# Pair loads on SP wait for earlier pair loads, and pair 0's block sums stand one slot later

## The reference

```python
k_sum = k.reshape(B, H, nb, block, D).max(axis=3)
v_sum = v.reshape(B, H, nb, block, D).mean(axis=3)
scores_l = scale * np.matmul(q, k.transpose(0, 1, 3, 2))      # kept where |i - j| < 16
scores_s = scale * np.einsum('bhsd,bhnd->bhsn', q, k_sum) + np.log(block)
a = softmax over both; return np.matmul(a, np.concatenate([v, v_sum], axis=2))
```

## Time and profile before

| What | Value |
|---|---|
| Median of 3 runs | 351.02 us (348.58 to 351.9) |
| Profiled execution, whole time | 350.21 us |
| Profiled execution, span | 348.3 us |
| PE busy | 337.7 us, 97% of the span |
| PE weight loads busy | 304.0 us, 87% |
| DVE, ACT, POOL busy | 61%, 35%, 34% |
| Data moved | 24.72 MB, mean 71 GB/s |
| Mean granted clock of PE | 0.99 |

### The profile page before, as it was taken

The page is one execution under the profiler, slowest core; times in us unless marked ns, Lnnn a source line. Parts: engine busy times, 40 slices in busy tenths (PEclk is TensorE's granted clock), DMA queues, the critical chain, the costliest instruction groups (busy, mean ns, idle before and its releaser), DMA issues.

```text
span 348.3 us, 7109 instructions
## 1 busy us (share of the span) xinstructions
PE 337.7 (97%) x2886; PEld 304.0 (87%) x2886; DVE 211.6 (61%) x503; ACT 123.2 (35%) x364; POOL 117.6 (34%) x130
## 2 busy tenths in 40 slices
PE   7879799999999999999999999999999999999996
PEld 6768688888998899889999999998999999999984
DVE  5658678434309990363447984688656667766652
ACT  3667677756233132451111124221222232222212
POOL 6557668856609999400004920000000000000000
PEclk9989899999999999999999999999999999999999
DMA  7999738000212200163000200000000004000004
GB/s 245 291 313 236 212 122 289 2 2 3 64 58 93 105 0 2 48 203 114 0 0 2 60 0 3 0 2 0 0 2 0 0 2 181 0 2 0 0 3 181
DMA packets 9024, 24.72 MB, mean 71 GB/s; under 512 B 1184, under 2 KB 1184, under 8 KB 8992
## 3 DMA queue, kind: packets, MB, share of 16 engines
q1 hardware_dynamic: 8992, 24.26, 22.4%
HBM read 21.11 MB, written 3.15 MB: 70 GB/s over the span
## 4 chain that ended last, share of the span: by engine, by line
PE 92%; DMA 2%; POOL 2%; issue 1%; ACT 1%; DVE 1%; SPq 0%; POOLq 0%; DVEq 0%
PE bank L799 26%; PE bank L800 26%; PE bank L801 26%; PE bank L791 4%; PE bank L778 3%; PE bank L758 3%; DMA vw<-in_vw 2%; PE bank L849 1%; PE bank L768 1%; POOL vw L393 1%; ACT P L505 1%; POOL P L421 1%; PE bank L852 1%; DMA out<-obuf 1%; PE bank L884 1%
## 5 line engine op out<-in xcount | busy, mean ns | idle before, releaser
L801 PE MATMUL bank<-g_h,W_l 128*128 128x384 f32 x128 | 43.0, 336 | 0.0
L800 PE MATMUL bank<-g_l,W_h 128*128 128x384 f32 x128 | 42.9, 335 | 0.0
L799 PE MATMUL bank<-g_h,W_h 128*128 128x384 f32 x128 | 42.9, 335 | 0.0
L505 ACT ACTIVATE P<-P,nmax 128x120 f32<-128x120 f32 x96 | 36.7, 384 | 15.5 <-DVE nmax L634 15.3
L801 PE MATMUL bank<-wo_h,hg_l 128*128 128x512 f32 x96 | 38.0, 396 | 0.0
L800 PE MATMUL bank<-wo_l,hg_h 128*128 128x512 f32 x96 | 38.0, 396 | 0.0
L799 PE MATMUL bank<-wo_h,hg_h 128*128 128x512 f32 x96 | 37.9, 395 | 0.0
L801 PE MATMUL bank<-wsT_h,vn_l 128*128 128x384 f32 x96 | 32.1, 334 | 0.0
L799 PE MATMUL bank<-wsT_h,vn_h 128*128 128x384 f32 x96 | 32.1, 334 | 0.0
L800 PE MATMUL bank<-wsT_l,vn_h 128*128 128x384 f32 x96 | 32.1, 334 | 0.0
L421 POOL TENSOR_TENSOR P<-P,rinv 128x480 f32<-128x480 f32 x24 | 23.6, 986 | 23.8 <-DVE rinv L622 23.4
(11 more groups left out here) (111 smaller groups left out, 798.0 us busy)
## 6 DMA issues: line engine op xcount, KB each, us to landing
vw<-in_vw SPq DMA_DIRECT2D x16, 288.0 KB, 6.1
kT<-in_k SPq DMA_DIRECT2D x8, 384.0 KB, 5.4
qT<-in_q SPq DMA_DIRECT2D x8, 384.0 KB, 6.4
out<-obuf SPq DMA_DIRECT2D x12, 256.0 KB, 2.0
stage<-in_wsT SPq DMA_DIRECT2D x6, 384.0 KB, 3.2
stage<-in_w SPq DMA_DIRECT2D x4, 512.0 KB, 3.5
stage<-in_wo SPq DMA_DIRECT2D x4, 512.0 KB, 3.5
wi_most<-in_w_in SPq DMA_DIRECT2D x3, 512.0 KB, 12.0
```

The source lines that it names most:

```text
L505: a.activation(P[:, i % NP_, j, :], P[:, i % NP_, j, :], ACT.Exp, bias=nmax[:, c:c + 1], scale=-1.0, accum_out=rsum[:, c, 0:1]).then_inc(e ...
L799: t_.matmul(dst, lhs[0](c), rhs[0](c), start=first, stop=False)
L800: t_.matmul(dst, lhs[0](c), rhs[1](c), start=False, stop=False)
L801: ins = t_.matmul(dst, lhs[1](c), rhs[0](c), start=False, stop=last)
```

## The change

The first part moves pair 0: its `vs` stands in slot 1 instead of slot 0, its `vp` in slot 2 instead of 1, on ACT ahead of slot 2's exponentials, and POOL spreads its sums after the normalisation of group 1 instead of group 0. The second adds waits on SP for the landing of an earlier load, from pair 2 on: kT of pair p waits for qT of pair p-1, qT for vw of pair p-1, vw for kT of pair p, and the rows of `w_in` for qT of pair p.

```diff
         for p in range(NP):
-            at = GP * p - 1 if p >= 2 else 3 * p
+            at = GP * p - 1 if p >= 2 else 3 if p == 1 else 1
             fills_at[at].append(("vs", p))
             fills_at[at + 1].append(("vp", p))
...
             for p in range(NP):
+                if p >= 2:
+                    sp.wait_ge(q_in[(p - 1) % NQB], 16 * ((p - 1) // NQB + 1))
                 load_k(p)
+                if p >= 2:
+                    sp.wait_ge(v_in[(p - 1) % NVB], 32 * ((p - 1) // NVB + 1))
                 load_q(p)
+                if p >= 2:
+                    sp.wait_ge(k_in[p % NQB], 16 * (p // NQB + 1))
                 load_v(p)
                 if 2 <= p < 2 + KC:
+                    sp.wait_ge(q_in[p % NQB], 16 * (p // NQB + 1))
                     load_wi(p - 2)
...
-                pool.wait_ge(norm_done, GP * p + 2 if p == 1 else GP * p + 1)
+                pool.wait_ge(norm_done, GP * p + 2 if p < 2 else GP * p + 1)
...
-                if i in (1, 5) or i >= 2 * GP and i % GP == 1:
+                if i in (2, 5) or i >= 2 * GP and i % GP == 1:
                     spread_sums(i // GP)
...
+                if i == 2:
+                    take(("vp", 0))
                 if i < NG:
                     for j in range(GT):
...
                 for u in fills_at[i]:
-                    if u[0] != "piece":
+                    if u[0] != "piece" and u != ("vp", 0):
                         take(u)
```

## The result

The changed kernel has a median of 345.37 us in 4 runs (343.85 to 346.16), beside 349.83 us of the kernel before (4 runs). The ratio is 0.9891 (0.9844 to 0.9938). A later comparison on another chip gave 0.9902 (0.987 to 0.9934), 344.70 against 347.70 us. The forecast was 342.0 us, 8.2 less than the profiled execution's 350.21; the changed kernel's profiled execution took 346.16, 4.05 less, and its median is 4.46 under the one before.

A forecast was written before the change was run, and what follows sets the result against it. PE was taken to bound the kernel, stopped twice by late instruction packets with a slow clock behind. Terms -1.2 (Part 1) - 4.1 - 3.3 (the stops) + 0.4 (waits) = -8.2 from 350.2 gave 342.0 us, range 340 to 349.5.

The forecast's parts named there:

- What bounds the kernel, and the stops: PE bounds the span; twice before 46 us it stops for a late instruction packet, 2.10 and 1.81 us, slow clock following.
- The 2.8 us of delay taken for a packet: Lateness assumed for instruction packets with the waits on SP, under the 3.3 us that stay hidden; bounds 0.1 and 5.7.
- Rival (b): Packet delay comes from busy DMA engines, not queue depth; neither stop goes, only Part 1 counts: 349.0 us; chance 0.15.
- Part 1: Pair 0's block sums a slot later: slot 4's scores at 15.15 against 16.36 us, gain 1.2 us, bounds 0 and 1.4.
- Part 2: Waits on SP for earlier loads, from pair 2 on: both instruction stops go, 4.1 and 3.3 us gained, 0.4 lost.
- The second stop: PE's instruction stop ending at 40.76 us, in slots 11 and 12: its removal with the slow clock gains 3.3 us.
- The first stop: PE's instruction stop from 20.28 us, in slots 5 and 6: its removal with the slow clock gains 4.1 us.
- what the waits may cost: vw of pair 2 landing after its block sums want it at 18.3 us: 0.4 us lost, bounds 0 and 1.3.
- rival (c): The load chain starves PE at pair 2 and pairs 3 to 5: slower, 358.8 us at 7 us per load; chance 0.10.
- Supply of the later pairs: Loads take 6 to 7 us a pair, three slots last 7.5, so supply stays ahead; other waits priced at nothing.
- rival (a): One instruction stop stays, or both at half, as the room is only 0.5 us: 345.7 us; chance 0.20.

The follow-up runs named there:

- three loads open for pair 2: Changed kernel with pair 2's loads waiting three places ahead, those from pair 3 on two; median 343.39 us, ratio 0.9869 to the kernel before.
- pair 2 free: Changed kernel with the loads of pair 2 and the first w_in rows issued without waits, waits from pair 3 on; 344.06 us, ratio 0.9913 to before.

## Why the prediction was wrong

**What bounds the kernel, and the stops.** Right. PE drained a packet and waited for the next; without the waits on SP both stops return, with them a packet of the changed kernel starts 0.9 to 4.4 us late and at most 0.40 us of stop is left (0.82 in one profile of the waits alone). The 2.8 us of delay taken for a packet fits: the mean over the changed kernel's two profiles is 2.6. Rival (b) said that neither stop goes and the time is 349.0; both went. That busy engines, rather than a deep queue, are what delays a packet is not refuted, since they were less busy too.

**Part 1, 1.2 us.** Measured 1.46 at slot 4, by the route described: scores 1 at 6.86, ScalarE idle 0.63 us ahead of slot 2's exponentials (0.7 forecast). The size rests on two profiles, and the start scatters: slot 4 came between 14.64 and 15.78 us in the profiles with the block sums moved and no stop ahead of it, and between 15.60 and 17.96 in those without the move. Missed was that this gain hangs on Part 2. With no waits the first packet's stop of 1.26 us takes it all; I had treated the two as a sum.

**The second stop, 3.3 us.** Measured 2.92; 0.40 of stop remained. Right, with its size.

**The first stop, 4.1 us, and what the waits cost, 0.4.** This is where the prediction failed. The stop did go. The term "what the waits may cost" was mis-sized: 0.4 was taken with a bound of 1.3, and slots 5 and 6 lost 9.02 - 5.26 = 3.8 us against the swap of vw and qT, which has no wait there. The instant at which PE wants the load was right (18.3 forecast; 20.47 - 2.37 = 18.1). The landing was wrong by 2.1 us (18.3 against 20.42), in three pieces. qT of pair 1 landed at 10.88, where I had 10.2. kT of pair 2 took 3.94 instead of 3.8. The second half of vw was issued at 15.22 behind the first and took 5.20, so vw needed 5.6 from the issue of the first; I had 4.3, though pair 5's halves already averaged 5.1. A part of this is chance: in three other profiles with the same waits vw of pair 2 landed at 19.31 to 19.55, inside the upper bound of 19.6. I took a short queue for an advantage, while it left the engines short (168 to 206 GB/s against 281 to 331). Then the price of a late load was counted as the wait alone, while the stretch at 1.2 GHz behind it was counted only in the sum of rival (c). The rows had shown that price at both stops: the idle time is about half of it.

The 4.1 us itself was a little too much. The 4.83 us needed for slots 5 and 6 came from slots without the warm-up transposes that slot 6 still holds; with no wait, the two take 5.23 to 5.29 us in three profiles, which leaves 3.6 to 3.7 for the stop and its slow clock.

**Supply of the later pairs, priced at nothing.** It had no lead to spare. In the changed kernel it held with PE already late; with vw of pair 2 ahead of its qT, pairs 3 and 4 came 1.33 and 1.60 us late, while with three loads open for pair 2 they were in time. Rival (c) was the right mechanism for pair 2, with the wrong size.

**Luck.** The median of 345.37 us lies in the forecast range and beside the 345.7 of rival (a). That is chance: (a) says that one stop for instructions stays, and none over 0.40 us did; a late load and its slow clock cost about as much.

**The base.** The profiled execution of before, 350.21 us with a mean clock of 0.99, was a slow specimen: later medians of this kernel were 347.55, 348.2 and 347.70 us, and one of its runs took 345.08. The mean clock of each execution tells roughly how many slow stretches it had: 0.99 with two in the profile of before, 0.995 with one in that of the changed kernel, 0.998 or more in the profiles without. Of 71 later executions of before, 20 were at 0.990 or below, 39 at 0.993 to 0.995 and 12 at 0.998 or more; these 12 took 345.08 to 348.08 us. So most executions had one slow stretch and not the two that the 8.2 us count on; a term read from one profile, where the rest of the runs lie below it, is an upper value for the median. Of the changed kernel's ten executions five had one, and of seven with pair 2 free and six with three loads open for it none was below 0.997.

**Open.** Why kT of pair 5 took 7.8 us in the changed kernel with so few loads open, and why the lateness of neighbouring packets scatters, is not settled. Nor is what sets the start: the wait for vw of pair 0 was between nothing and 1.68 us. How many executions of before have both stops is known only by their clock, since a stop without a slow stretch leaves no trace in it.

## What to carry to other kernels

Where an engine stands still with nothing missing, look for an instruction packet on the DMA queues at that time, and count instructions to see when it was due: a deep queue of loads can be what it waits for. A limit on open loads is a trade: with two open the packets came in sooner here and the rate fell, with three the rate held and most packets were late again. The best median came with the limit of two set behind the urgent loads, though not clear of the noise. And price a wait of PE with the slow clock that may follow: at 1.75 to 2.4 us of idle the whole cost was 1.6 to 1.85 times the idle.

## What the runs showed of the hardware

Pair 1's kT, qT and vw landed at 9.3, 10.7 and 12.9 us with pair 2's loads queued behind them, and at 9.1, 10.9 and 12.9 without. Over all profiles qT landed at 10.5 to 10.7 with them (three) and at 9.9 to 11.0 without (nine). So loads did not clearly delay those ahead of them in their own queue, while without a limit the instruction packets of another queue were 2.2 to 6.5 us late.

Idle of PE of 0.40 to 1.33 us, for instructions or for a load, left the clock at 1.00; that of 1.68 to 2.37 us came with a stretch at 0.50. In between it went either way: 1.54 us at 39.1 and 1.60 at 36.6 were not followed by it, 1.57 at 33.3 and 1.52 near the start (8.26 us) were.
